# A gated linear scan with two mixture-of-experts layers: the scan stage worked one chunk deeper

## What is computed

```python
sig_r, sig_i = sigmoid(r_gate), sigmoid(i_gate)
a_t = exp(8 * sig_r * log(clip(sigmoid(a_param), 1e-6, 1 - 1e-6)))
norm = sqrt(maximum(1 - a_t * a_t, 1e-6))
x_gated = norm * sig_i * x
for t in range(S):
    h = a_t[:, t] * h + x_gated[:, t]
    y[:, t] = h
```

## Time and profile before

| what | value |
|---|---|
| median of three runs | 1464.65 us |
| profiled execution | 1465.98 us, span 1464.5 |
| TensorE / VectorE / ScalarE / GpSimd busy | 1286.9 / 838.4 / 728.7 / 464.5 us |
| mean granted clock of TensorE | 0.905 |
| first stage | from 0 to about 227 us of the span |
| first stage, scan inputs 2 to 10 | 48.20 to 213.77 us, eight stages |

### The profile page before, as it was taken

One profiled execution on the slowest core, in us unless ns is written; L12 is line 12 of the kernel. 1 busy time (PEld: TensorE's weight loads), 2 busy tenths in 40 slices (PEclk: granted clock), 3 DMA queues, 4 the chain that ended last, 5 costly groups with the idle time before them and its releaser, 6 DMA issues. The chain is left out here.

```text
span 1464.5 us, 28375 instructions
## 1 busy us (share of the span) xinstructions
PE 1286.9 (88%) x9338; PEld 1196.4 (82%) x9340; DVE 838.4 (57%) x2271; ACT 728.7 (50%) x1347; POOL 464.5 (32%) x585
## 2 busy tenths in 40 slices
PE   3656657887599999999999999489999999999997
PEld 3655656666259999999999999479999999999997
DVE  5778777666746665665666666534335444435332
ACT  5555644455327675666666666334334344334332
POOL 3344530000034444443444444322222222222222
PEclk9788766566779999999999999789999999999999
DMA  6566732210021231222223221252213331311111
GB/s 216 184 180 210 228 120 83 87 58 30 1 79 59 74 101 41 101 70 69 72 73 102 73 73 44 72 177 76 70 39 98 102 106 48 98 43 42 43 43 43
DMA packets 81201, 129.16 MB, mean 88 GB/s; under 512 B 7974, under 2 KB 63919, under 8 KB 81104
## 3 DMA queue, kind: packets, MB, share of 16 engines
q1 hardware_dynamic: 62448, 74.10, 15.9%
q0 software_dynamic: 18656, 53.81, 11.6%
HBM read 94.61 MB, written 35.10 MB: 89 GB/s over the span
## 5 line engine op out<-in xcount | busy, mean ns | idle before, releaser
L972 PE MATMUL ps<-xTh,w1h 128*128 128x256 f32 x1312 | 376.4, 287 | 5.3 <-issue 3.5
L976 PE MATMUL ps<-xTl,w1h 128*128 128x256 f32 x1312 | 372.9, 284 | 0.2 <-issue 0.2
L973 PE MATMUL ps<-xTh,w1l 128*128 128x256 f32 x1312 | 372.8, 284 | 0.0
L1569 DVE SCALAR_TENSOR_TENSOR hidl<-ps,hidh 128x512 fp32r<-128x512 f32 x328 | 225.7, 690 | 230.5 <-ACT hidh L696 221.8
L696 ACT ACTIVATE hidh<-ps 128x512 fp32r<-128x512 f32 x328 | 195.5, 596 | 250.9 <-PE ps L976 242.3
L972 PEld LDWEIGHTS ps<-xTh,w1h 128*128 128x128 f32 x1312 | 252.5, 192 | 6.3 <-issue 3.9
L973 PEld LDWEIGHTS ps<-xTh,w1l 128*128 128x128 f32 x1312 | 252.8, 193 | 1.7
L976 PEld LDWEIGHTS ps<-xTl,w1h 128*128 128x128 f32 x1312 | 253.0, 193 | 0.4 <-issue 0.4
L1009 PE MATMUL ps<-w2hl,hidh 128*128 128x512 f32 x672 | 239.9, 400 | 0.0
L993 PE MATMUL ps<-w2hl,hidh 128*128 128x264 f32 x640 | 185.1, 289 | 0.0
L995 PE MATMUL ps<-w2hl,hidl 128*128 128x264 f32 x640 | 182.1, 285 | 0.0
(11 more groups left out here) (280 smaller groups left out, 2266.7 us busy)
## 6 DMA issues: line engine op xcount, KB each, us to landing
w1st<-in_moe_w_dram SPq DMA_DIRECT2D x20, 1024.0 KB, 5.5
w2st<-in_moe_w_dram SPq DMA_DIRECT2D x19, 1024.0 KB, 5.5
xrow<-y_rows POOLq DMA_DIRECT2D x44, 258.0 KB
arena<-in_r_gate_dram SPq DMA_DIRECT2D x19, 512.0 KB, 4.8
arena<-in_i_gate_dram SPq DMA_DIRECT2D x19, 512.0 KB, 5.9
arena<-in_x_dram SPq DMA_DIRECT2D x19, 512.0 KB, 6.7
h_rows<-w2st POOLq DMA_DIRECT2D x19, 512.0 KB, 4.2
y_rows<-arena SPq DMA_DIRECT2D x8, 258.0 KB, 2.7
```

The source lines that it names most:

```text
L972: pe.matmul(o, wh, xTh[:, hf, :], start=(hf == 0), stop=False)
L973: pe.matmul(o, wl, xTh[:, hf, :], start=False, stop=False)
L976: mm = pe.matmul(o, wh, xTl[:, hf, :], start=False, stop=(hf == HB - 1))
L1569: dve.scalar_tensor_tensor(out=hidl[:, 2 * fp:2 * fp + 2, :].rearrange("p c t -> p (c t)"), in0=bank(fp), scalar=0.0, in1=hidh[:, 2 * fp:2 ...
```

## The change

- Rows are turned and copied two chunks later than their inputs are transposed, in place of one: stage s handles the rows of chunk s-2, in one block of eight tiles between its two input halves, on TensorE, VectorE and GpSimd.
- The root of chunk s-1 is taken on ScalarE between the two halves of chunk s, in place of at the end of stage s-1.
- The squares move from GpSimd to ScalarE, two behind each half. GpSimd keeps only the stores.
- One copy of 272 columns takes a tile's rows and logits as they lie in the bank; `row_copied` now frees the bank. The buffer is wider for it (`w2room`). One addition per chunk (`logits`) adds the halves of the logits for eight tiles. Since the buffer holds the two channel blocks apart, a store is two DMAs with pieces of 512 bytes in DRAM, in place of one with pieces of 1024.
- Bounds handle both channel blocks of a half at once, two a chunk.
- The scan input of chunk s-1 comes behind the first half of chunk s on VectorE.
- The constants are made ahead of the first chunk.

The loop over chunks now has four stages written out ahead of it in place of two. The core of the diff:

```diff
-        w2st = sb("w2st", [P, FC, D], F32)
+        RW = P + E
+        w2room = sb("w2room", [P, max(FC * D, 2 * LOAD * HB * RW)], F32)
+        w2st = w2room[:, 0:FC * D].rearrange("p (c d) -> p c d", d=D)
...
-        rowbuf = w2st[:, :, :].rearrange("p (b t) d -> p b t d", b=2)
+        rowbuf = w2room[:, 0:2 * LOAD * HB * RW].rearrange("p (t h c) -> p t h c", h=HB, c=RW)
...
-            def square(s, par, j, n, hf):
-                pool.wait_ge(decay_done, units_before(s) + j * HB + hf + 1)
-                a = a_sb[:, par, hf, j * LW:j * LW + n * P]
-                pool.tensor_tensor(q_sb[:, par, hf, j * LW:j * LW + n * P], a, a, ALU.mult
-                                   ).then_inc(square_done, 1)
-
             def store_rows(s, j, n):
-                pool.wait_ge(row_copied, CHUNK * s + LOAD * j + n)
-                pool.dma_start(h_rows[ds(s * CW + j * LW, n * P), :].rearrange("(t p) d -> p t d", p=P),
-                               rowbuf[:, j, 0:n, :]).then_inc(rows_stored[j], 16)
+                pool.wait_ge(row_copied, CHUNK * s + LOAD * j + n + 2)
+                for h in range(HB):
+                    pool.dma_start(h_rows[ds(s * CW + j * LW, n * P), h * P:(h + 1) * P].rearrange(
+                        "(t p) c -> p t c", p=P), rowbuf[:, LOAD * j:LOAD * j + n, h, 0:P]).then_inc(rows_stored[j], 16)
...
+                if not (isinstance(s, int) and s < 2):
+                    for j in range(2):
+                        store_rows(s - 2, j, LOAD)
...
+                for hf in range(HB):
+                    act.wait_ge(decay_done, u(hf) + 1)
+                    act.activation(q_sb[:, par, hf, c0:c0 + w], a_sb[:, par, hf, c0:c0 + w], ACT.Square
+                                   ).then_inc(square_done, 1)
...
+            def norm(s, par, tiles):
+                w = tiles * P
+                act.wait_ge(q_done, 2 * (s + 1))
+                act.activation(q_sb[:, par, :, 0:w], q_sb[:, par, :, 0:w], ACT.Sqrt, scale=-0.25
+                               ).then_inc(n_done, 1)
...
-                for j, n in loads(tiles):
-                    for hf in range(HB):
-                        unit(s, par, j, n, hf)
-                w = tiles * P
-                act.wait_ge(q_done, units_before(s) + HB * len(loads(tiles)))
-                act.activation(q_sb[:, par, :, 0:w], q_sb[:, par, :, 0:w], ACT.Sqrt, scale=-0.25
-                               ).then_inc(n_done, 1)
+                (j0, n0), (j1, n1) = loads(tiles)
+                half(s, par, j0, n0)
+                if not (isinstance(s, int) and s == 0):
+                    norm(s - 1, 1 - par, CHUNK)
+                half(s, par, j1, n1)
 
             chunks(act, stage)
+            norm(NS - 1, (NS - 1) % 2, tiles_of[-1])
...
+                for j, n in loads(tiles):
+                    for hf in range(HB):
+                        turn_inputs(s, j, n, hf)
+                    if j == 0 and not (isinstance(s, int) and s < 2):
+                        rows_and_logits(s - 2, CHUNK)
...
+            later_constants()
...
-            def bound(s, par, j, n, hf):
+            def bound(s, par, j, n):
 
                 c0, w = j * LW, n * P
-                dve.wait_ge(square_done, units_before(s) + j * HB + hf + 1)
-                dve.tensor_scalar(q_sb[:, par, hf, c0:c0 + w], q_sb[:, par, hf, c0:c0 + w], 1.0, -1e-6,
+                dve.wait_ge(square_done, units_before(s) + j * HB + HB)
+                dve.tensor_scalar(q_sb[:, par, :, c0:c0 + w], q_sb[:, par, :, c0:c0 + w], 1.0, -1e-6,
                                   ALU.subtract, ALU.min).then_inc(q_done, 1)
...
-            def copy_rows(s, first, last):
-                for t in range(first, last):
+            def copy_rows(s, tiles):
+                for t in range(tiles):
                     tt = CHUNK * s + t
-                    j = t // LOAD
                     dve.wait_ge(row_T, tt + 1)
-                    if t % LOAD == 0 and not (isinstance(s, int) and s == 0):
-                        dve.wait_ge(rows_stored[j], 16 * s)
-                    both = bank(6 + t % 2)[:, 0:HB * (P + E)].rearrange("p (h c) -> p h c", h=HB)
-                    dve.tensor_copy(rowbuf[:, j, t % LOAD, :].rearrange("p (h c) -> p h c", h=HB),
-                                    both[:, :, 0:P]).then_inc(row_copied, 1)
-                    dve.tensor_reduce(L[:, ds(tt, 1), :].rearrange("p o e -> p (o e)"),
-                                      both[:, :, P:P + E].rearrange("p h e -> p e h"), AX.X, ALU.add
-                                      ).then_inc(row_free, 1)
+                    if not (isinstance(s, int) and s == 0):
+                        if t == 0:
+                            dve.wait_ge(logits_made, s)
+                        if t % LOAD == 0:
+                            dve.wait_ge(rows_stored[t // LOAD], 32 * s)
+                    dve.tensor_copy(rowbuf[:, t, :, :].rearrange("p h c -> p (h c)"), bank(6 + t % 2)[:, 0:HB * RW]
+                                    ).then_inc(row_copied, 1)
+
+            def logits(s, tiles):
+                dve.wait_ge(row_copied, CHUNK * s + tiles + 2)
+                dve.tensor_tensor(L[:, ds(CHUNK * s, tiles), :], rowbuf[:, 0:tiles, 0, P:RW], rowbuf[:, 0:tiles, 1, P:RW],
+                                  ALU.add).then_inc(logits_made, 1)
 
             def stage(s, par, tiles):
-                units = [(j, n, hf) for j, n in loads(tiles) for hf in range(HB)]
-                earlier = not (isinstance(s, int) and s == 0)
-                if earlier:
+                (j0, n0), (j1, n1) = loads(tiles)
+                known = isinstance(s, int)
+                for hf in range(HB):
+                    gate(s, par, j0, n0, hf)
+                if not (known and s < 2):
+                    copy_rows(s - 2, CHUNK)
+                bound(s, par, j0, n0)
+                if not (known and s < 2):
+                    logits(s - 2, CHUNK)
+                if not (known and s == 0):
                     scan_input(s - 1, 1 - par, CHUNK)
                 for hf in range(HB):
-                    gate(s, par, *units[hf])
-                    if earlier:
+                    gate(s, par, j1, n1, hf)
+                    if not (known and s == 0):
                         scan_half(s - 1, 1 - par, CHUNK, hf)
-                for k, unit in enumerate(units):
-                    if k >= HB:
-                        gate(s, par, *unit)
-                    bound(s, par, *unit)
-                    if earlier and k == max(len(units) - 2, HB - 1):
-                        copy_rows(s - 1, 0, LOAD)
-                if earlier:
-                    copy_rows(s - 1, LOAD, CHUNK)
-                else:
-                    later_constants()
+                bound(s, par, j1, n1)
 
             chunks(dve, stage)
+            copy_rows(NS - 2, tiles_of[-2])
+            logits(NS - 2, tiles_of[-2])
             scan_input(NS - 1, (NS - 1) % 2, tiles_of[-1])
             for hf in range(HB):
                 scan_half(NS - 1, (NS - 1) % 2, tiles_of[-1], hf)
-            copy_rows(NS - 1, 0, tiles_of[-1])
-
-
-
-            dve.wait_ge(row_free, NT + 2)
+            copy_rows(NS - 1, tiles_of[-1])
+            logits(NS - 1, tiles_of[-1])
```

More of the change, by code:

```diff
@@ L342, in chunks @@
             tiles = [min(CHUNK, NT - CHUNK * s) for s in range(NS)]
-            pairs = max(0, (sum(t == CHUNK for t in tiles) - 2) // 2)
-            for s in range(min(2, NS)):
+            pairs = max(0, (sum(t == CHUNK for t in tiles) - 4) // 2)
+            for s in range(min(4, NS)):
                 stage(s, s % 2, tiles[s])
@@ L347, in chunks @@
                 with eng.Fori(0, pairs) as i:
-                    stage(2 * i + 2, 0, CHUNK)
-                    stage(2 * i + 3, 1, CHUNK)
-            for s in range(2 + 2 * pairs, NS):
+                    stage(2 * i + 4, 0, CHUNK)
+                    stage(2 * i + 5, 1, CHUNK)
+            for s in range(4 + 2 * pairs, NS):
                 stage(s, s % 2, tiles[s])
@@ L410, in load_folds @@
                     if i == 1:
+                        sp.wait_ge(logits_made, NS)
                         for j in range(2):
-                            sp.wait_ge(rows_stored[j], 16 * sum(len(loads(t)) > j for t in tiles_of))
+                            sp.wait_ge(rows_stored[j], 32 * sum(len(loads(t)) > j for t in tiles_of))
                     elif i > 1:
@@ L791, in turn_inputs, with rows_and_logits @@
                     mm.then_inc(done, 1)
-            def rows_and_logits(s, first, last):
+            def rows_and_logits(s, tiles):
                 pe.wait_ge(scan_done, 2 * s + 4)
-                for t in range(first, last):
-                    pe.wait_ge(row_free, CHUNK * s + t + 1)
+                for t in range(tiles):
+                    pe.wait_ge(row_copied, CHUNK * s + t + 1)
                     for hf in range(HB):
-                        mm = pe.matmul(bank(6 + t % 2)[:, hf * (P + E):(hf + 1) * (P + E)],
```

(12 more changed lines are left out.)

45 lines of the change are left out of this document (20 added, 25 removed).

## The result

The changed kernel takes 1446.89 us in the median of four runs (1442.35 to 1450.42), against 1464.59 for the kernel before: a ratio of 0.988, interval 0.985 to 0.992. That is 17.7 us less, where 27.1 were forecast; the time lies in the range, 9.4 us above the forecast. The profiled execution took 1445.22 us, its span is 1443.8.

A forecast was written before the change was run, and what follows sets the result against it. VectorE sets the pace, with 15.97 us of work and 4.7 of waits a stage. Seven stages of 17.3 us give -24.8, start +1.3, end -3.7: -27.2 us, to 1437.5 us; range 1426 to 1449.

The forecast's parts named there:

- VectorE's work: VectorE's busy time in a first-part stage falls from 15.97 to 13.9 us through reduces, copies, logits, bounds and scans.
- the wide bounds: On VectorE, four bounds of 512 become two of 1024 at the double pace: -1.3 us a stage, at least 0.1.
- VectorE's waits: VectorE waits only in the block of row copies, 1.9 or 4.2 us a stage, plus 0.2 for signals.
- my own walk: Step-by-step timing of one stage across engines: scans and bound until 6.1 us, first-half gates until 7.3, then eight copies.
- the forecast's own signs: Expected in the profile: stages of 16 to 18.3 us, VectorE idle 2 to 4 us before copies, none before gates and bounds.
- The block of copies: Eight row copies on VectorE, paced by TensorE: 4.8 us at the full clock, 7.1 at the low; one clock fall a stage.
- rival 1: TensorE stays at the low clock through the whole block of copies: 18.3 us a stage, 1446 us; chance 0.18.
- ScalarE: ScalarE gets four squares of 512 and is busy 13.6 to 14.4 us a stage, under the stage's 17.3.
- Each us late would cost a us: ScalarE's root lies 4 us and its squares 6 us early; without that cover, each us late lengthens the stage equally.
- The DMA rival: DMA engines become the bound through 512-byte store pieces: 18 to 19 us a stage, about 1448 us; chance 0.05.
- Start: Constants moved to the front are hidden, but chunk 0's scan input comes later: second scan input at 49.5 us, +1.3.
- End: From the ninth scan input to the last logits, 28.9 us in place of 32.6: -3.7.

The follow-up runs named there:

- the first experiment: The changed kernel with ScalarE's wait for the scan of chunk s-2 moved from ahead of the first tanh to ahead of the exponentials: 1425.27 us, ratio 0.973.
- both edits: The changed kernel with ScalarE's wait moved ahead of the exponentials and spare matmuls in TensorE's pauses (4, not 14, behind the scan): 1421.04 us, ratio 0.970.

## Why the prediction was right and where it was wrong

**VectorE's work.** 13.9 us forecast, 14.0 measured. The bounds of 1024 take 0.68 us and hold the engine 0.60 (105.76 to 106.36 us in the timeline), as taken; the Trainium skill's rule on the double pace (VectorE: DVE Perf Modes, Mode 2×_2P) is borne out for two blocks of 512. The quiet scan takes 2.34 us, 2.32 was scaled from the last chunk. The logits take 0.22 us and hold the engine 0.14. The 1.3 us that the forecast gave to the wide bounds came, but little of it from the width: four quiet bounds of 512 would hold VectorE 4 x 0.34 = 1.36 us and two wide ones hold it 1.20. Most of the old cost stood beside GpSimd's squares, where two bounds of the kernel before took 2.37 us and a quiet one 0.41:

```profile
176.29 7.19 POOL L472 TENSOR_TENSOR arena<-arena 128x512 f32<-128x512 f32 x3 [1.69 <-ACT arena L619]
...
181.39 2.37 DVE L1157 TENSOR_SCALAR arena<-arena 128x512 f32<-128x512 f32 x2
...
184.28 0.41 DVE L1157 TENSOR_SCALAR arena<-arena 128x512 f32<-128x512 f32 x1
```

In the changed order a bound waits for both squares of its half, and with the squares back on GpSimd it still took 0.67 us. No run changes the width alone.

**VectorE's waits, the step that failed.** "VectorE makes the two gates of the first half until 7.3 without a wait: ScalarE has had its tanh by 3.6." ScalarE had not, because its stage begins with the wait for the scan of chunk s-2. Before, that scan ended in the first half of stage s-1, and ScalarE's tanh waited for TensorE and never for a scan (69.2 us in rows 4); with the scans moved behind the first half it ends last on VectorE, where my own walk had put it, at 5.4. I walked TensorE past `scan_done` but left ScalarE's wait on the same semaphore out. It costs 11.5/7 = 1.64 us a stage directly, and 2.42 with the clock that it keeps down: the first experiment gets back 21.6 us, more than the whole 9.4 between forecast and result. Two of the forecast's own signs said so: no wait before the gates, and a stage of 18.3 us at most. Neither came.

**The block of copies.** The granted clock falls once in each of the seven stages. In three of them it is 0.50, which is 1.2 of 2.4 GHz, from the first tile to the last (58.09 to 67.55 us, 95.60 to 105.16, 150.94 to 160.36). In the other four it is 0.58 to 0.67 over the last six tiles, so low for a part of them. The forecast had one fall a stage that ends within the block: so it was in four, and rival 1 describes the other three. Rival 1 was held unlikely because each pause is under 2.2 us. That was no protection: in four stages the clock was down at the first two tiles (0.50 to 0.53), after pauses of 1.31 and 1.60 to 1.69 us with 0.66 us of matmuls between them. Of the block the waits are 20.0/7 = 2.9 us, where 3.1 lay in the middle of 1.9 and 4.2 (the middle of the two stages, 16.0 and 18.3, is 17.15 and not 17.3, 1 us in all). The near match has some luck in it. The pauses were longer than in the walk, as the gate waits held up the copies and TensorE stood still for 1.7 to 2.8 us before its third tile; without these waits the mean clock is 0.86 in place of 0.79. And a tile at the low clock costs the block 0.91 us, not 1.0 to 1.09. Rival 1 gave 1446, which is nearly the measured time, but not for its reason: it had 18.3 us a stage from a block of 7.1 us, and the block is about 6.2 (118.20 to 123.83 us in one stage, 5.6, and 99.07 to 105.76 in another, 6.7), with 1.64 us of gates beside it.

**ScalarE.** 13.6 to 14.4 forecast, 94.36/7 = 13.5 measured; a square takes 0.64 us (0.63 was taken). VectorE waited for no root in these stages. "Each us late would cost a us" was never tried, since it was not late.

**GpSimd and DMA.** The stores take 20.1% of 129.88 us, 3.7 us a stage (3.4 to 5 was taken), and land after 3.0 us. The DMA engines are busy 0.69 of the time, and 0.86 at 270 GB/s with both edits; in neither does TensorE wait for input in the seven stages. The DMA rival falls. In the same seven stages the stores of the kernel before, with pieces of 1024 bytes, took 16.7% of 145.89 us, 3.5 us a stage, so pieces of 512, in twice as many DMAs, cost 7% more. That they cost so little agrees with the least size in the Trainium skill (DMA: Bandwidth & Descriptors, Specifications).

**Start.** +1.3 forecast, +1.85 measured; the gates of chunk 2 met the same wait (0.57 and 0.98 us). That the constants are hidden in front was right: the first gate starts at 14.65 us with them there and at 14.63 with them behind chunk 0. Where they stood in the kernel before they were not hidden.

**End.** -3.7 forecast, from 32.6 to 28.9; measured 27.3 (179.93 to 207.26). The 15 tiles were turned faster than taken, in 6.3 and 5.7 us.

**The sum.** -24.8 for seven stages was -16.0, +1.3 was +1.85, -3.7 was -5.3: -27.2 against -19.4 in the profiles, and 17.7 between the medians. The time fell into the range because the range reached to the low clock, not because it knew the wait; that is luck, and 2 us more would have left it.

## What to carry to other kernels

When a step is moved, list every wait on its semaphore, on all engines, and ask at what time each is now released: a guard for a buffer that cost nothing starts to pace an engine when the step it names moves to the end of the stage. Put such a guard in front of the one instruction that needs it. And where an engine's clock depends on its work, time the block that follows a pause at the low clock, and remove the pause before shortening what stands beside it: 0.4 us less work a stage in a block that another engine paces was worth nothing that the times could tell.

## What the hardware showed that was not expected

- An operation on two columns, the mask, takes 0.22 us in the changed kernel (L1177) and 1.00 us in each of its four instances when GpSimd squares beside it (L1184; in one stage the mask starts at 108.24 us and GpSimd's two squares run from 107.56 to 110.23). Being tiny does not spare it; the scans, 2.49 in place of 2.34 us in the mean, lose less.
- After 44 spare products (2.6 us) and a pause of 4.48 us the clock over the next eight tiles was 0.71, as with 12, while 8, 12 and 14 spare products (0.6, 0.8 and 1.0 us), spread over a stage's three pauses, kept the mean clock at 0.99.
